# Gate logits on two engines and another order of experts, in a fused attention and two-MoE kernel

## The reference

```python
x = attention(q, k, v)                  # 64-token chunks, 8 heads of 64; x is (2304, 512)
p = domain_probs / (domain_probs.sum(-1) + 1e-9)
for e in range(4):                      # first MoE: every token through every expert
    y += p[:, e] * (relu(x @ w1[e]) @ w2[e])          # 512 -> 1024 -> 512
logits = y @ w_gate                     # (2304, 8)
expert = argmax(logits); gate = softmax(logits)[expert]
for e in range(8):                      # second MoE: each token through one expert
    out[expert == e] = gate * (relu(y[expert == e] @ v1[e]) @ v2[e])
```

## Time and profile before

| | |
|---|---|
| median of three runs | 1233.73 us (1231.23 to 1233.78) |
| the profiled execution | 1234.42 us |
| its span, first to last instruction | 1232.6 us |
| mean granted TensorE clock | 0.994 |
| attention and first expert's first five groups | about 0 to 262 us |
| gated groups g = 1 to 4 | about 725 to 877 us |
| second MoE, from block 0's second product | about 933 us to the end |
| transfers | 81.11 MB, 66 GB/s over the span |

### The profile page before, as it was taken

How to read it: one execution, slowest core, us unless ns; L and a number is a source line. 1 busy time by engine, 2 the same in 40 slices (tenths; PEclk the granted TensorE clock), 3 DMA queues, 4 the chain that set the end, 5 groups by cost and what they waited for, 6 DMA issues and landing times.

```text
span 1232.6 us, 18555 instructions
## 1 busy us (share of the span) xinstructions
PE 1207.6 (98%) x6388; PEld 1070.5 (87%) x6389; DVE 462.6 (38%) x939; ACT 267.2 (22%) x416; POOL 315.5 (26%) x192
## 2 busy tenths in 40 slices
PE   8999999999999999999999999999998999999986
PEld 6999999999999999999999998899985888888875
DVE  4432442432222222222222223334356555555543
ACT  1222222223111113211112311122133011131420
POOL 7300000006000005100001500101047853185892
PEclk9999999999999999999999999999998999999998
DMA  9322112013000003000001200000273441272730
GB/s 245 78 52 55 47 51 60 9 49 97 1 0 0 0 0 119 17 0 0 0 0 59 77 26 27 1 25 26 79 181 118 123 149 72 68 249 73 252 129 21
DMA packets 92639, 81.11 MB, mean 66 GB/s; under 512 B 48255, under 2 KB 72959, under 8 KB 92610
## 3 DMA queue, kind: packets, MB, share of 16 engines
q1 hardware_dynamic: 84594, 67.88, 18.5%
q0 software_dynamic: 4416, 11.30, 3.0%
q10 hardware_dynamic: 3600, 1.57, 0.6%
HBM read 71.12 MB, written 10.92 MB: 67 GB/s over the span
## 4 chain that ended last, share of the span: by engine, by line
PE 91%; issue 2%; POOL 2%; DMA 2%; DVE 1%; ACT 1%; POOLq 0%; SPq 0%; DVEq 0%; ACTq 0%
PE psum L1135 14%; PE psum L1137 14%; PE psum L1136 14%; PE psum L1166 10%; PE psum L1168 10%; PE psum L1167 10%; PE psum L1338 3%; PE psum L1063 3%; PE psum L1340 3%; PE psum L1339 3%; PE psum L1080 3%; POOL weights_r L417 2%; PE psum L1325 1%; PE psum L1185 1%; DMA weights<-in_moe_w 1%
## 5 line engine op out<-in xcount | busy, mean ns | idle before, releaser
L417 POOL TENSOR_TENSOR weights_r<-weights,weights_r 128x1024 fp32r<-128x1024 f32 x96 | 232.1, 2443 | 678.6 <-ACT weights_r L570 677.8
L1135 PE MATMUL psum<-xhi,weights_r 128*128 128x384 f32 x768 | 261.0, 340 | 1.1 <-DVEq L724 0.4
L1137 PE MATMUL psum<-xhi,weights_r 128*128 128x384 f32 x768 | 257.0, 335 | 0.0
L1136 PE MATMUL psum<-xlo,weights_r 128*128 128x384 f32 x768 | 256.8, 334 | 0.0
L1166 PE MATMUL psum<-weights_r,hhi 128*128 128x512 f32 x576 | 228.7, 397 | 0.0
L1168 PE MATMUL psum<-weights_r,hlo 128*128 128x512 f32 x576 | 225.1, 391 | 0.0
L1167 PE MATMUL psum<-weights_r,hhi 128*128 128x512 f32 x576 | 224.5, 390 | 0.0
L730 DVE SCALAR_TENSOR_TENSOR hlo<-psum,hhi 128x384 fp32r<-128x384 f32 x192 | 106.9, 557 | 262.8 <-ACT hhi L565 262.8
L565 ACT ACTIVATE hhi<-psum 128x384 fp32r<-128x384 f32 x192 | 94.5, 492 | 510.8 <-PE psum L1137 510.3
L1135 PEld LDWEIGHTS psum<-xhi,weights_r 128*128 128x128 f32 x768 | 144.3, 188 | 4.3 <-DVE xlo L691 2.2
L1136 PEld LDWEIGHTS psum<-xlo,weights_r 128*128 128x128 f32 x768 | 144.3, 188 | 0.7
(11 more groups left out here) (172 smaller groups left out, 1147.8 us busy)
## 6 DMA issues: line engine op xcount, KB each, us to landing
weights<-in_moe_w SPq DMA_DIRECT2D x96, 512.0 KB, 5.4
qT<-in_q SPq DMA_DIRECT2D x36, 128.0 KB, 3.1
x_rows<-xfin SPq DMA_DIRECT2D x18, 256.0 KB, 2.3
kT<-in_k SPq DMA_DIRECT2D x15, 256.0 KB, 3.4
vbd<-in_v SPq DMA_DIRECT2D x30, 128.0 KB, 2.8
kT<-in_k ACTq DMA_DIRECT2D x3, 256.0 KB, 4.3
vbd<-in_v ACTq DMA_DIRECT2D x6, 128.0 KB, 7.3
meta<-slot_table SPq DMA_DIRECT2D x25, 1.0 KB, 2.5
```

What stands on the lines that cost most here:

```text
L417: gp.tensor_tensor(rounded(set_, 1, c), raw(set_, c), rounded(set_, 0, c).bitcast(F32), ALU.subtract).then_inc(sem("w_lo"), 1)
L1135: mm(out_, ahi, bhi, start=(i == 0), stop=False)
L1136: mm(out_, ahi, blo, start=False, stop=False)
L1137: last = mm(out_, alo, bhi, start=False, stop=(i == n - 1))
```

## The change

The kernel gets a second copy of the gate matrix, transposed (`gate_rows`, 8 x 512), which SP broadcasts to all partitions in the space of the attention's inputs when the attention is over. In the four passes of the loop, the logits of tiles 1 and 2 are computed on DVE: for each of the eight experts one multiplication of the tile's finished rows with the expert's gate row, with a running sum over the 512 columns into one element of `lg`. Four buffers for the products (which nobody reads) are used in turn, with a wait for the product four back. Tile 1's eight products stand behind the low halves of f = 0 to 5, tile 2's behind that of f = 7, and its choice now stands ahead of the next group's low input. PE keeps transposes and logits for tile 0 alone; the rank products stay for all three, tile 2's after output step 6 instead of 4. ACT copies only tile 0's transposes. The last group and the tail gate as before, with their semaphore counts renumbered (`nth`).

In the order of experts, place = min(2 * rank, 15 - 2 * rank): ranks 0, 7, 1, 6, 2, 5, 3, 4.

```diff
+    wg_row = tile("wg_row", [P, E2, D], F32, a0)
+    product = tile("product", [P, 4, D], F32, a0 + 4 * E2 * D)
...
+    lg = small("lg", [P, TG - 1, E2], F32)
...
+    ROW_LOGITS = [[0], [1, 2], [3], [4], [5, 6], [7], [], []]
+
+    def nth(t):
+
+        return TP // TG + t - TP
...
             sp.wait_ge(sem("o_psum"), NT)
+            sp.dma_start(wg_row[:, :, :], gate_rows.unsqueeze(0).to_broadcast([P, E2, D])).then_inc(sem("wg_row_in"), 16)
...
                     if gated is not None:
-                        if f in (1, 5):
-                            take_gT(gated * TG + f // 4, G_B[f // 4])
+                        if f == 1:
+                            take_gT(gated, G_B[0])
+                        if f == 5 and last:
+                            take_gT(gated + 1, G_B[1])
...
                 if gated is not None:
-                    take_gT(gated * TG + 2, G_B[2])
+                    if last:
+                        take_gT(gated + 2, G_B[2])
                     gate_exp(gated * TG + 2)
...
+            def row_logits(g, i, experts):
+
+                for e in experts:
+                    if e > 3:
+                        dve.wait_ge(sem(f"row_logit{i}"), (g - 1) * E2 + e - 3)
+                    vec.scalar_tensor_tensor(product[:, e % 4, :], xfin[:, i, :], 1.0, wg_row[:, e, :], ALU.mult, ALU.mult,
+                                             accum_out=lg[:, i - 1, e:e + 1]).then_inc(sem(f"row_logit{i}"), 1)
+
+            def choose(t, i, bank, k=None, g=None):
+
+                if g is None:
+                    dve.wait_ge(sem("logit_psum"), (nth(t) if k is None else k) + 1)
+                    logits = psum[:, bank, 0:E2]
+                else:
+                    dve.wait_ge(sem(f"row_logit{i}"), g * E2)
+                    logits = lg[:, i - 1, :]
...
+            dve.wait_ge(sem("wg_row_in"), 16)
+
             def gated_group(g):
 
                 t = (g - 1) * TG
+                dve.wait_ge(sem("y_taken"), (E1 - 1) * NT + g * TG + 1)
                 for f in range(FT):
                     take_hlo(n0 + g, f)
-                    if f in (2, 6):
-                        choose(t + f // 4, f // 4, G_B[f // 4])
-                    if f in (3, 7):
-                        assign(t + f // 4, G_B[f // 4])
+                    if f == 2:
+                        choose(t, 0, G_B[0], k=g - 1)
+                    if f == 3:
+                        assign(t, G_B[0])
+                    if f == 6:
+                        choose(t + 1, 1, None, g=g)
+                    if f == 7:
+                        assign(t + 1, G_B[1])
+                    row_logits(g, 1, ROW_LOGITS[f])
+                row_logits(g, 2, range(E2))
+                choose(t + 2, 2, None, g=g)
                 take_xlo(n0 + g + 1, g + 1)
-                choose(t + 2, 2, G_B[2])
                 assign(t + 2, G_B[2])
                 for i in range(TG):
-                    dve.wait_ge(sem("g_psum"), t + i + 1)
+                    if i == 0:
+                        dve.wait_ge(sem("g_psum"), g)
                     take_y(n0 + g, E1 - 1, g, i, final=True)
...
-                vec.tensor_scalar(swap[:, :], rank_, -2.0, 16.0, ALU.mult, ALU.add)
-                then(vec.tensor_scalar(place_, rank_, 2.0, -1.0, ALU.mult, ALU.add), "order_step", 4)
+                vec.tensor_scalar(swap[:, :], rank_, -2.0, float(2 * E2 - 1), ALU.mult, ALU.add)
+                then(vec.tensor_scalar(place_, rank_, 2.0, None, ALU.mult), "order_step", 4)
+                vec.tensor_tensor(place_of[:, :], place_, swap[:, :], ALU.min)
                 then(vec.tensor_tensor(place_, place_, swap[:, :], ALU.min), "order_step", 5)
-                then(vec.tensor_scalar(place_of[:, :], place_, 0.0, None, ALU.max), "order_step", 6)
-                vec.tensor_scalar(place_, place_, 0.0, None, ALU.max)
...
             with pe.Fori(1, NG - 1) as g:
                 t = (g - 1) * TG
                 for f in range(FT):
                     hidden(E1 - 1, n0 + g, f)
-                    gate(t + f // 4, f // 4, f % 4, (1, 2, 3))
+                    gate(t, 0, f, (1, 2, 3), k=g - 1)
+                    if f == 7:
+                        rank(t + 1, G_B[1])
                 for f in range(FT):
                     output(E1 - 1, n0 + g, f)
-                    gate(t + 2, 2, f, (0, 2, 4))
+                    if f == 6:
+                        rank(t + 2, G_B[2])
```

More of the change, by code:

```diff
@@ L3, with chunked_attention_then_two_moes @@
 from contextlib import ExitStack
-def chunked_attention_then_two_moes(nc, q, k, v, domain_probs, w1, w2, w_gate, v1, v2, out):
+def chunked_attention_then_two_moes(nc, q, k, v, domain_probs, w1, w2, w_gate, gate_rows, v1, v2, out):
     F32, F32R, BF16 = mybir.dt.float32, mybir.dt.float32r, mybir.dt.bfloat16
@@ L570, in split_hi, with take_gT @@
                 sc.activation(rounded(set_, 0, c), raw(set_, c), ACT.Copy).then_inc(sem("w_hi"), 1)
-            def take_gT(t, bank):
-                act.wait_ge(sem("g_psum"), t + 1)
+            def take_gT(k, bank):
+                act.wait_ge(sem("g_psum"), k + 1)
                 sc.activation(gT[:, :, :], psum[:, bank, :].rearrange("x (r t) -> x r t", r=KT), ACT.Copy)\
@@ L579, in gate_exp, with group @@
                 sc.activation(lshift[:, :], lshift[:, :], ACT.Exp, accum_out=lsum[:, :]).then_inc(sem("lsum_ready"), 1)
-            def group(n, following=None, first=None, after=None, gated=None, t0=None):
+            def group(n, following=None, first=None, after=None, gated=None, t0=None, last=False):
                 for f in range(FT):
@@ L625, in _ @@
                 group(n0 + g, g + 1, gated=g - 1)
-            group(LAST, after=E1 + 1, gated=NG - 2)
+            group(LAST, after=E1 + 1, gated=NG - 2, last=True)
             for i in range(TG - 1):
-                take_gT(NT - TG + i, G_B[i])
+                take_gT(nth(NT - TG + i), G_B[i])
                 gate_exp(NT - TG + i)
-            take_gT(NT - 1, G_B[TG - 1])
+            take_gT(nth(NT - 1), G_B[TG - 1])
             split_hi(0, E1 + 1, NW // 2)
@@ L772, in _ @@
                         take_y(e * NG + g, e, g, i)
-            def choose(t, i, bank):
-                dve.wait_ge(sem("logit_psum"), t + 1)
-                logits = psum[:, bank, 0:E2]
+            def row_logits(g, i, experts):
[11 more added lines that the diff above has]
+                    logits = lg[:, i - 1, :]
                 vec.tensor_copy(topf[:, :], logits[:, 0:1])
@@ L839, in order_experts @@
                 then(vec.reduce_sum(rank_, cells, axis=X), "order_step", 3)
-                vec.tensor_scalar(swap[:, :], rank_, -2.0, 16.0, ALU.mult, ALU.add)
-                then(vec.tensor_scalar(place_, rank_, 2.0, -1.0, ALU.mult, ALU.add), "order_step", 4)
+                vec.tensor_scalar(swap[:, :], rank_, -2.0, float(2 * E2 - 1), ALU.mult, ALU.add)
+                then(vec.tensor_scalar(place_, rank_, 2.0, None, ALU.mult), "order_step", 4)
+                vec.tensor_tensor(place_of[:, :], place_, swap[:, :], ALU.min)
                 then(vec.tensor_tensor(place_, place_, swap[:, :], ALU.min), "order_step", 5)
-                then(vec.tensor_scalar(place_of[:, :], place_, 0.0, None, ALU.max), "order_step", 6)
-                vec.tensor_scalar(place_, place_, 0.0, None, ALU.max)
[L847 to L850, removed]
+                then(vec.tensor_scalar(swap[:, :], place_of[:, :], 2.0, float(8 * E2), ALU.is_ge, ALU.mult), "order_step", 6)
+                then(vec.tensor_tensor(cells, col(ids), row(place_), ALU.is_equal), "order_step", 7)
+                then(vec.tensor_tensor(cells, cells, row(ids), ALU.mult), "order_step", 8)
+                then(vec.reduce_sum(at_, cells, axis=X), "order_step", 9)
                 vec.tensor_copy(expert_at[:, :], at_).then_inc(sem("order_ready"), 1)
@@ L873, in take_last @@
             def take_last(i):
-                dve.wait_ge(sem("g_psum"), t + i + 1)
+                dve.wait_ge(sem("g_psum"), nth(t + i) + 1)
                 take_y(n0 + g, E1 - 1, g, i, final=True)
@@ L1180, in transpose_x, with logits @@
                 last.then_inc(sem("g_psum"), 1)
-            def logits(t, bank):
-                pe.wait_ge(sem("gT_ready"), t + 1)
+            def logits(k, bank):
+                pe.wait_ge(sem("gT_ready"), k + 1)
                 for kt in range(KT):
@@ L1214, in _, with gate @@
             pe.wait_ge(sem("wg_in"), 16)
-            def gate(t, i, f, at_steps):
+            def gate(t, i, f, at_steps, k=None):
                 if f == at_steps[0]:
@@ L1220, in gate @@
                 if f == at_steps[1]:
-                    logits(t, G_B[i])
+                    logits(nth(t) if k is None else k, G_B[i])
                 if f == at_steps[2]:
@@ L1279, in _ @@
             first_block(0, [2])
-            logits(NT - 1, G_B[TG - 1])
+            logits(nth(NT - 1), G_B[TG - 1])
             first_block(0, [3]).then_inc(sem("l1a_psum"), 1)
@@ L1394, in _ @@
```

(6 more changed lines are left out.)

## The result

The changed kernel takes 1218.97 us (median of four, 1218.22 to 1219.54) against 1232.48 for the kernel before: ratio 0.9887, 95% interval 0.9866 to 0.9908. The forecast was 1220.5, range 1218 to 1225.5. All runs compared here are fast ones.

A forecast was written before the change was run, and what follows sets the result against it. TensorE (PE), busy 98% of the span, sets the time, except one stall on POOL. 9.3 + 4.3 = 13.6 us off the profiled 1234.42 gives 1220.8, stated as 1220.5 because that execution lay 0.7 above the median; range 1218 to 1225.5.

The forecast's parts named there:

- the rank wait: Gated loop: PE reaches tile 1's rank before DVE has chosen, losing 0.42 us a group, 1.7 us in all.
- Gate work off PE: Gated loop: PE loses transposes and logits of two tiles a group, 1.375 us each; 8 tiles give 11.0 us.
- three of four: Groups in the change's name; the prediction read all four from the diff; with three the term would be 8.3 us.
- Part 1: Gate logits moved to DVE in the four-group loop: 11.0 - 1.7 = 9.3 us gained.
- The product: DVE's 128x512 multiplication with running sum in the gated loop: 0.76 us each, between 0.59 and 0.94.
- The fit: DVE's 2.96 + 4p between low halves f = 3 and f = 6, against PE's 6.35 us: fits to p = 0.85.
- Rival A: DVE's accumulating product is slow, 1.14 us; part 1 gains only 4.7 us, 1225.4; chance 0.17.
- The other covers: DVE's work elsewhere in the loop stays hidden; additions into xfin end at most 0.5 us later than now.
- The new transfer: SP's 2 MB broadcast of gate rows before the second expert's weight loads: cost zero.
- The order: Second MoE: the new order of experts removes PE's one stall on POOL, 16.54 - 12.25 = 4.3 us.
- Rival B: Second MoE: the stall moves to another single block instead of going; order gains 0, 1225.1; chance 0.11.
- Rival C: Gated loop: DVE becomes the bound; gain used up at 1.55 us a product, 1239 at 1.65; chance 0.05.

The follow-up runs named there:

- double products: Changed kernel with each of DVE's 16 products per group done twice, the first into a place nobody reads: 1223.43 us, ratio 0.9924.
- threefold products: Changed kernel with each of DVE's 16 products per group done three times: 1256.98 us, ratio 1.0194.
- the order alone: Kernel before with only the new order of experts: 1228.65 us, ratio 0.9968.
- the order that rises: Changed kernel with experts ordered largest first, then from the smallest up (6, 1, 1, 1, 2, 2, 4, 6 blocks): 1235.13 us, ratio 1.0022.
- gate alone: Changed kernel with the old order of experts: 1222.59 us, ratio 0.9914.
- the later rank: Changed kernel with tile 1's rank products one PE step later, behind output step f = 0: 1218.29 us, ratio 0.9884.
- both with three tiles: Changed kernel with all three loop tiles' logits on DVE: tile 0's rank behind hidden f = 5, 1214.13 us; behind f = 6, 1212.95 us.

## Why the prediction was right, step by step

The forecast of 1220.5 was 1.5 us too high, and 1.25 of this is the reference: it was taken off a median of 1233.73 for the kernel before, and the four runs that the ratio uses have 1232.48. In the profiles, 13.6 us were forecast and 14.8 measured. Of this 1.2, the rank wait is 0.75. The rest lies in stages that the forecast left alone, and is chance as far as the runs show.

- **Gate work off PE, 11.0 us.** Groups went from 37.65 to 35.15 us. With the lost 0.25 us of the rank wait added back, 2.75 us a group are gone from PE, 11.0 in all. There are 64 products, 16 in each of four groups: the name's "three of four" is not what the code does.
- **The rank wait, 1.7 us.** The mechanism was right, the size was not: 0.22 to 0.25 us a group, 1.0 in all, inside the bounds that I gave. The term that was too large is the 0.43 us from DVE's start of "chosen" to the weight load. It came from the earlier trace rows, where that load had been idle for 0.27 us. But 0.26 us stand in front of a load behind output products even where PE waits for nothing (792.60 above), so those rows hold no wait that could be priced. Where PE does wait in the loop, the load starts 0.28 to 0.29 us behind the start of "chosen" (777.83 and 778.12), and it is the same with doubled and threefold products (793.12 and 793.41). "Chosen" starts 1.32 us behind the low half of f = 6 (1.34 expected), and PE would have been there at 1.36: 1.32 + 0.29 - 1.36 = 0.25. Part 1 was 10.05 us, not 9.3; this term is the difference.
- **The product, 0.76 us.** It is 0.61. I put the readout of 0.10 on top of 0.66 from start to start, but it takes no place of its own; and the 0.66, from additions that read PSUM, was itself 0.05 more than these products need. The fit is up to p = 0.94 rather than 0.85 (the low half with an assignment is 1.74 us, the others 0.47 from start to start, not 0.56). With double products, at 1.22, this arithmetic gives 1.1 us; the low half of f = 3 was already 0.1 late there, and the measured cost is 1.20.
- **Rival A, the slow product.** The Trainium skill, "Vector Engine (DVE) Microarchitecture Reference", section "Points that are easy to get wrong", has this form at half rate when both sources are in SBUF and not bf16. The trace of after does not agree: 512 columns took 0.69 us with both sources float32 in SBUF. Half of the rate at which the earlier trace rows has the low x (0.59 us for 512 columns) would be an estimated 1.18.
- **The other covers** held: low x was done 6.6 us before the next group (786.42 + 1.76, against 794.8), PE waited for DVE at no other place of the loop. xfin was done 1.8 us into the next group, 2.4 before PE needs it; that is 0.6 later than in the kernel before, where I had allowed 0.5.
- **The new transfer, zero.** It took 7.0 us to land, and the next one was issued 8.9 us behind it.
- **The order, 4.3 us.** It is 4.3 us in the profiles, and 2.5 to 5.4 by the times of the order alone. Rival B did not come: none of the single blocks stalled PE. That the stall is POOL's throughput (19 us an expert and the stores) and not the arrival of the weights is shown by the order that rises, where POOL works for 58.7 us without a break and PE waits for it; the 16.6 us are its pace of 19.9 us an expert and of 4.7 us for the two low halves of half a matrix.
- **Rival C** is real and where it was put: a product of three times the length makes the kernel slower than before. Its sum left out TensorE's clock, which made 2.1 of the 9.3 us that each group lost. Its turning point of 1.55 us was not tried by itself; 1.22 and 1.84 lie on either side.

Open: from the last addition of the loop to R(0) the kernels took 78.1 us (before), 76.9 (after), 77.8 (order alone), 77.9 (gate alone) and 76.5 (rising order). The others reach from 77.5 to 79.3. So the 0.7 us that after gained there lie within what the stretch varies by, and nothing is read from them. PE stands still several times in this stretch and its mean granted clock is 0.94 to 0.98 there, so part of the spread may be the clock; that was not tested. And in five of the ten profiled executions (after, the later rank, the double products, both with three tiles) the blocks stood 12.29 us apart, in the other five 12.25, at the same granted clock of 1.00. The kernel with threefold products has after's order, and its blocks are 12.25 us apart. The difference makes 0.5 us in all, and its cause is open.

## What to carry to other kernels

Ask of the engine that takes work over not how busy it is on average but whether the work fits between two of its deadlines: with the products doubled, one stretch of three PE steps was too short and cost 1.2 us a group. And where the critical engine is TensorE, a long wait can cost more than itself, since the clock behind it was halved. When work leaves the critical engine, that engine arrives sooner at its next wait, so move that wait on by a step in the same change. Work that a slower engine must do once per expert (19 us here) hides behind long experts and not behind short ones, so alternate them.

## What the runs showed of the hardware

A float32 multiplication of two SBUF operands with a running sum takes 0.69 us for 128x512, its readout 0.08, and back to back they come every 0.61 us, no slower than the same tile added from PSUM (0.66 to 0.75). I had left room for half that rate. A 2 MB broadcast of 16 KB to all partitions lands in 7.0 us, some 300 GB/s. TensorE's weight load starts 0.28 to 0.29 us behind the start of the 0.23 us VectorE instruction that it waits for, in every wait of the gated loop. And TensorE's granted clock fell to 0.50 while the engine stood still for 4.96 us (threefold products) and 6.77 us (rising order) and stayed there for 4.6 and 2.7 us of work after the wait; around a wait of 1.64 us (doubled products) it was 1.00.
